# Weight loads of 64 columns in place of 128 for two groups of small TensorE products in a linear-attention and mixture-of-experts kernel

## The reference

```python
def phi(x):
    proj = np.einsum('bhsd,df->bhsf', x, w_phi)
    proj = proj - np.max(np.abs(proj), axis=-1, keepdims=True)
    return np.concatenate([np.exp(proj), np.exp(-proj)], axis=-1)
q_p, k_p = (phi(q), phi(k))
kv = np.einsum('bhsf,bhsd->bhfd', k_p, v)
z = np.sum(k_p, axis=2)
num = np.einsum('bhsf,bhfd->bhsd', q_p, kv)
den = np.einsum('bhsf,bhf->bhs', q_p, z)[..., None] + 1e-06
return (num / den).astype(np.float32)
```

## Time and profile before

| | |
|---|---|
| median of three runs | 1611.26 us |
| the profiled execution's own time | 1612.77 us |
| its span | 1610.9 us |
| TensorE busy | 1541.6 us (96%) |
| VectorE, ScalarE, GpSimd busy | 805.0, 601.0, 436.1 us |
| attention loop | the first 505 us or so |
| granted TensorE clock, mean | 0.98 of full speed |

### The profile page before, as it was taken

One profiled execution on the slowest core, in us unless ns is written; L12 is line 12 of the kernel. 1 busy time (PEld: TensorE's weight loads), 2 busy tenths in 40 slices (PEclk: granted clock), 3 DMA queues, 4 the chain that ended last, 5 costly groups with the idle time before them and its releaser, 6 DMA issues. The chain is left out here.

```text
span 1610.9 us, 32416 instructions
## 1 busy us (share of the span) xinstructions
PE 1541.6 (96%) x9650; PEld 1302.3 (81%) x9650; DVE 805.0 (50%) x1530; ACT 601.0 (37%) x1025; POOL 436.1 (27%) x434
## 2 busy tenths in 40 slices
PE   6999999999998999999899999969999999999996
PEld 5888888888887888888788888757888788788885
DVE  3777677677776543233444323446422352454431
ACT  4666666666653322122332212232211331333220
POOL 2121221231363322332233233134222222222221
PEclk9999999999999999999999999978999999999998
DMA  5333333333731521111323111133411242442210
GB/s 125 80 89 79 78 83 80 79 80 82 226 95 35 210 93 41 40 38 38 124 82 104 41 41 40 57 109 132 151 47 41 89 147 92 142 151 88 86 52 26
DMA packets 180956, 141.50 MB, mean 88 GB/s; under 512 B 131243, under 2 KB 150059, under 8 KB 180272
## 3 DMA queue, kind: packets, MB, share of 16 engines
q1 hardware_dynamic: 157440, 92.67, 19.5%
q0 software_dynamic: 19936, 46.42, 8.9%
q10 hardware_dynamic: 3408, 0.10, 0.1%
HBM read 105.92 MB, written 32.67 MB: 86 GB/s over the span
## 5 line engine op out<-in xcount | busy, mean ns | idle before, releaser
L1451 PE MATMUL bank<-wts,xh 128*128 (+1 forms) x640 | 260.3, 407 | 17.1 <-DVE wts L779 9.9
L1463 PE MATMUL bank<-wts,hh 128*128 (+1 forms) x640 | 260.1, 406 | 5.2 <-DVE hl L1134 2.7
L1453 PE MATMUL bank<-wts,xl 128*128 (+1 forms) x640 | 253.3, 396 | 0.0
L1452 PE MATMUL bank<-wts,xh 128*128 (+1 forms) x640 | 253.1, 395 | 0.0
L1464 PE MATMUL bank<-wts,hh 128*128 (+1 forms) x640 | 251.4, 393 | 0.9 <-issue 0.9
L1465 PE MATMUL bank<-wts,hl 128*128 (+1 forms) x640 | 251.9, 394 | 0.0
L703 ACT ACTIVATE hh<-bank 128x512 fp32r<-128x512 f32 x160 | 86.9, 594 | 331.7 <-PE bank L1501 326.4
L1115 DVE TENSOR_SCALAR hid<-bank 128x512 f32<-128x512 f32 x80 | 55.3, 691 | 265.4 <-PE bank L1453 262.0
L1127 DVE TENSOR_SCALAR ys<-bank,pair 128x512 f32<-128x512 f32 x80 | 60.0, 750 | 230.1 <-PE bank L1465 223.9
L1411 PE MATMUL p_n<-kvs,qp 128*128 128x100 f32 (+1 forms) x1280 | 162.5, 278 | 3.6 <-ACT kvs L608 1.0
L1411 PEld LDWEIGHTS p_n<-kvs,qp 128*128 128x128 f32 (+1 forms) x1280 | 143.8, 182 | 21.2 <-ACT kvs L608 10.1
(11 more groups left out here) (260 smaller groups left out, 2496.8 us busy)
## 6 DMA issues: line engine op xcount, KB each, us to landing
raw<-in_moe_w SPq DMA_DIRECT2D x52, 1024.0 KB, 9.9
qs<-in_q SPq DMA_DIRECT2D x64, 128.0 KB
ks<-in_k SPq DMA_DIRECT2D x64, 128.0 KB
vs<-in_v SPq DMA_DIRECT2D x64, 128.0 KB
x_tokens<-xo SPq DMA_DIRECT2D x32, 256.0 KB, 2.9
wts<-raw POOLq DMA_DIRECT2D x4, 1024.0 KB, 4.7
xin<-x_tokens,pair POOLq DMA_INDIRECT x86
bins<-pair,idx POOLq DMA_INDIRECT x83
```

The lines of the kernel that those rows point to most:

```text
L1451: eng.matmul(dst[:, :], xh[:, c, :], wh, start=c == 0, stop=False)
L1452: eng.matmul(dst[:, :], xh[:, c, :], wl, start=False, stop=False)
L1453: last = eng.matmul(dst[:, :], xl[:, c, :], wh, start=False, stop=c == DC - 1)
L1463: eng.matmul(b_y[:, :], hh[:, c, :], wh, start=c == 0, stop=False)
```

## The change

Every product with 128 weight columns in `spread_kv` and in the main tiles of `numerator` becomes two products with 64 weight columns. The first of them takes the lower 64 columns and writes PSUM partitions 0 to 63, the second takes the upper 64 and writes partitions 64 to 127. Both stream the same 73 or 100 columns. The tail of a numerator, which had 64 weight columns already, is as before. Nothing else is altered; waits and signals stand on the same first and last product. Lines 1279 to 1412 of the kernel before are one or two higher in the changed one.

```diff
+HALF = 64
@@ spread_kv
                 for h in range(2):
                     for g in range(2):
                         n = 2 * h + g
-                        last = eng.matmul(p_k[:, n * XW:(n + 1) * XW], kvt[:, n * FEAT:(n + 1) * FEAT],
-                                          msel[:, (2 * i + h) % H, :], start=True, stop=True)
+                        for a in range(2):
+                            last = eng.matmul(p_k[HALF * a:HALF * (a + 1), n * XW:(n + 1) * XW],
+                                              kvt[:, n * FEAT + HALF * a:n * FEAT + HALF * (a + 1)],
+                                              msel[:, (2 * i + h) % H, :], start=True, stop=True)
@@ numerator
                 for c in range(CT):
-                    if c < MAIN:
-                        cols, m = slice((4 * h + c) * P, (4 * h + c + 1) * P), P
-                    else:
-                        cols, m = slice(8 * P + TAIL * h, 8 * P + TAIL * h + TAIL), TAIL
+                    at, halves = ((4 * h + c) * P, 2) if c < MAIN else (8 * P + TAIL * h, 1)
                     for g in range(2):
-                        last = eng.matmul(p_n[h][0:m, c * NW:(c + 1) * NW], qp[:, g, cols], kvs[:, h, g, :],
-                                          start=g == 0, stop=g == 1)
+                        for a in range(halves):
+                            last = eng.matmul(p_n[h][HALF * a:HALF * (a + 1), c * NW:(c + 1) * NW],
+                                              qp[:, g, at + HALF * a:at + HALF * (a + 1)], kvs[:, h, g, :],
+                                              start=g == 0, stop=g == 1)
```

## The result

The changed kernel takes 1587.9 us (median of four runs, 1586.67 to 1589.05); the kernel before, with one run more beside it, 1612.2 us. The ratio is 0.984, with a 95% interval of 0.980 to 0.988. The forecast was 1589 us. Kernels that were run later stood beside other medians of the kernel before (1600.6 to 1619.4 us), so runs of different groups are compared by their ratio to it and by the lengths of passes in their traces, which repeat to 0.01 us.

What follows compares the result with a forecast made beforehand. TensorE was taken to bound the attention loop, with ScalarE capping plain passes. Savings of 14.3, 5.3, 1.6 and 1.5 us sum to 22.7, taking 1612.8 to 1590.1, forecast as 1589 us by the median; range 1572 to 1604.

Steps and rivals of the forecast that it cites:

- Side by side, 0.087 us a pair: In a numerator, records of different column halves run together, one pair per 0.087 us step: 1.89 us, saving 0.56.
- rival 1: Numerator and spread pairs run together but held at 0.112 us by shared load path or issue: 1602 us; chance 0.14.
- Spread: Split `spread_kv` product early in each pass: eight pair steps at 0.065 us, 0.71 to 0.79 us, saving about 0.2.
- ScalarE's cap in a plain pass: In 22 plain passes `xq` cannot start before ScalarE's exponentials end, so only 0.65 us a pass arrives, 14.3 us.
- Routing passes: Seven passes working out routing positions: VectorE's chain moves with the first numerator's end, 0.76 us each, 5.3 us.
- The end of the loop: Two passes after the routing ones gain about 0.8 us each, 1.6; the last two numerators, not hidden, gain 1.5.
- rival 5: Gain partly lost to a clock fall once TensorE idles, or waits in the layers: 1595 to 1608 us; chance 0.09.
- Sum: Over the attention loop, plain passes, routing passes, the two after them and the last numerators together save 22.7 us.
- rival 4: All 43 us that TensorE saves over the loop arrive, ScalarE being no bound: 1570 us; chance 0.04.

Runs made afterwards that it cites:

- early `xq`: Changed kernel with ScalarE's copies `xq` and `xtt` moved ahead of the last two key exponentials: ratio 0.975 to the kernel before, median 1560.5 us.

## Why the prediction was right, point by point

**Side by side, 0.087 us a pair: right.** A numerator was to take 1.89 us and takes 1.86. That the order of the same products decides over 55 us shows it. The evidence for it was borrowed from row halves, and thinner than it was read: the two records of `shared_tile` differ in rows alone, not "in rows and columns". Both write PSUM partitions from 0 up, in two banks, and those shown have 65 weight columns, which no half holds. So no row spoke of column halves, and that they behave like row halves was a bet that came true. The Trainium skill ("TensorE: Matmul & The Clock Gate", Part 3, "Measured speedup vs the span model") gives 2.38x for three column tiles and so points the same way. The rule of the Trainium skill in the same Part 3 ("What overlaps and what doesn't") that a load overlaps with matmuls in flight only when the row group differs is refuted here: all records of a numerator use all 128 rows, and a pair of 64-column loads and matmuls is done every 0.086 us, less than one record's load takes (0.137).

**Issue is no bound at 0.112 (rival 1): right.** 36 records in 1.68 us between first and last start are 0.047 us a record.

**Spread: too low.** Forecast were 0.2 us. From its start to the transpositions it saves 0.30, and 0.38 reach the numerator. Two steps of the working failed. The sum has one pair step too many: eight pairs have seven steps, in the trace the first of 0.11 us and six of 0.063, not 0.14 and seven of 0.065 (the spread of rival 1 has the same slip). And what the numerator waits for is not the spread's place in TensorE's stream but ScalarE's copy `kvs` of its result, which starts behind the spread's last record. ScalarE before, then after:

```profile
303.05 0.42 ACT L608 ACTIVATE kvs<-p_k 128x292 f32<-128x292 f32 x1 [1.46 <-PE p_k L1366]
303.19 0.42 ACT L609 ACTIVATE kvs<-p_k 128x292 f32<-128x292 f32 x1 [1.09 <-PE p_k L1368]
```

In both kernels the numerator starts 0.05 us after this copy ends. The copy starts 1.15 us after the spread did before, and 0.77 now: 0.38 less, like the lengths of the spread's rows, 1.11 and 0.73 us. The change back to 128 columns does cost what was feared, about 0.1 us (0.16 us from the last pair to the first transposition, before 0.11; then 0.17, before 0.11), but the wait for `kvs` covers it.

**ScalarE's cap in a plain pass: right**, 0.68 us against 0.65, the value 0.67 by the start spacing rather than 0.57 by the idle time. The wait ahead of `shared_tile` is 0.86 us, forecast 0.9. Removing it gave 0.84.

**Routing passes: 0.76 forecast, 0.96 measured** in six of seven (15.40 to 14.45). VectorE's chain did start with the first numerator's end, and that came 0.96 earlier: 0.59 for the numerator and 0.38 for the spread by way of `kvs`. The wrong term is the spread's again.

**The end of the loop: wrong in its parts, right in the sum by luck.** Forecast were 0.8 for the seventh routing pass, 1.6 for the two after it with its like, and 1.5 for the last numerators. Measured: 1.6 us lost in the seventh, 1.6 won in the pass after it, 4.2 in what follows. The mechanism of rival 5, a fall of the clock once TensorE idles, did occur, in the seventh routing pass, behind the long step of VectorE. But a fall was also spared at the end, and nothing in the change is seen to have spared it: the waits ahead of the last two numerators are the same as before (1.21 and 0.52 us), and with early `xq`, which has the same numerators and the same waits, the clock fell there and they took 5.3 us. Timeline of PE, then the clock:

```profile
458.75 5.30 PE L1412 MATMUL p_n<-kvs,qp 128*64 128x100 f32 x72 [0.51 <-ACT kvs L609]
```

```profile
459.00:462.00 3.00, 3.00 (x39) 0.50 0.00 0
```

The one fall cost 1.6 us, the one spared gave some 1.7 (5.30 against 3.65 us). The forecast, which left the clock as it was, had neither.

**Sum.** Forecast 22.7 us for the loop. Measured 25.0 (the first expert tile at 479.78 instead of 504.77): plain passes 14.9, routing 5.7, the last three stretches 4.2, the first pass 0.4, less 0.1 by which the loop starts later. The layers behind gained 1.1 us more without a cause in the change. The 43 us of rival 4 did not arrive; the trace has what is missing as the longer wait for `xtt`.

## What to carry to other kernels

Weights of 128 columns with a short moving operand are bound by their load (a step of 0.112 us whether 100, 73 or 16 columns stream); split in two column halves that run side by side, a group takes three quarters of the time, if records of unlike halves stand close in the stream (here within four records). Before such a change, ask what waits at the engine next in line: here ScalarE's order let 0.68 of 1.5 us through, and moving two copies in its stream freed the rest. Shorter work also shortens the time that queued instructions cover for what stands behind them, such as register loads: the router lost more there than it had won.

## What the runs showed of the hardware

- Float32 records on different column halves start 6 or 7 ns apart (every other record in the changed kernel) and take one step of 0.086 us together. A lone record of 64 columns with 100 streamed takes the same 0.086.
- Order within a numerator: switching halves every 2 or every 4 records gives 1.93 us, every 8 records 2.16, once 3.02. A record started ahead of three of the other half: the first upper record began beside the fifth of eight, and the seventeenth of twenty.
- The router in halves, 64-column float32 products behind fp32r ones of 128 columns, starts 0.09 us later than the undivided one. From 64 columns back to transpositions of 128 costs about 0.1 us in the attention loop, half of it ahead of the first transposition and half behind it.
- A step of 0.19 us on VectorE took 0.27 to 1.45 us where it started while GpSimd ran a 4.6 us subtraction, and ended 0.06 or 0.07 us after it in all twelve traces. That it waits for the other to end is read from this; no run moved the subtraction away.
